# TensorE's program of a fused convolution and SwiGLU kernel: 28 written-out token tiles become a hardware loop over pairs of tiles

## The reference, cut to what matters

```python
def _attn_ref(x, weight_gen):               # x (4, 4096, 192), weight_gen (4, 4096, 8, 7)
    w = exp(weight_gen - max) ; w = w / (sum(w) + 1e-9)           # softmax over 7 taps
    x_unf = windows of 7 tokens of x, padded with 6 zero tokens in front
    return einsum('bshk,bskhg->bshg', w, x_unf)                   # 16384 tokens of 192

def _moe_ref(x, w_gate, w_val, w_out, rms_g):
    xn = x / sqrt(mean(x * x) + 1e-06) * rms_g
    g = xn @ w_gate                         # 192 x 1536
    silu = g * (1.0 / (1.0 + np.exp(-g)))
    val = xn @ w_val                        # 192 x 1536
    return (silu * val @ w_out)             # 1536 x 192
```

## Time and profile before

| | before |
|---|---|
| time, median of 3 (lowest, highest) | 1334.78 us (1332.74, 1336.92) |
| profiled execution, its own time | 1334.78 us |
| its span, first to last instruction | 1333.0 us |
| mean granted TensorE clock | 0.988 of full |
| TensorE busy, matmuls | 1280.2 us (96%), 13524 |
| VectorE busy | 995.2 us (75%) |
| ScalarE busy | 662.8 us (50%) |
| GpSimd busy | 97.1 us (7%) |

### The profile page before, as it was taken

How to read it: one execution, slowest core, us unless ns; L and a number is a source line. 1 busy time by engine, 2 the same in 40 slices (tenths; PEclk the granted TensorE clock), 3 DMA queues, 4 the chain that set the end, 5 groups by cost and what they waited for, 6 DMA issues and landing times.

```text
span 1333.0 us, 33644 instructions
## 1 busy us (share of the span) xinstructions
PE 1280.2 (96%) x13524; PEld 1230.0 (92%) x13524; DVE 995.2 (75%) x1438; ACT 662.8 (50%) x1427; POOL 97.1 (7%) x104
## 2 busy tenths in 40 slices
PE   3797899999999999999999999999999999999998
PEld 3686789999988889999999999999999999999998
DVE  6777867877777777777777777777777777777653
ACT  4364464455554455554445555445555544555543
POOL 7701200000000000000000000000000000000000
PEclk9798899999999999999999999999999999999999
DMA  9121111122112212212112211211221211121010
GB/s 306 35 67 25 50 58 55 37 67 67 49 60 64 57 37 66 66 43 66 54 40 63 66 58 51 66 55 37 66 66 43 66 55 52 52 66 34 16 37 13
DMA packets 20101, 77.69 MB, mean 58 GB/s; under 512 B 3215, under 2 KB 5007, under 8 KB 19854
## 3 DMA queue, kind: packets, MB, share of 16 engines
q1 hardware_dynamic: 19982, 75.83, 19.0%
HBM read 38.07 MB, written 12.58 MB: 38 GB/s over the span
## 4 chain that ended last, share of the span: by engine, by line
PE 91%; DVE 3%; ACT 2%; issue 2%; DMA 1%; POOL 0%; SPq 0%; POOLq 0%
PE up_ps L619 59%; PE out_ps L650 24%; PE out_ps L654 7%; DVE h L545 1%; DMA xT<-xT 1%; DVE prod L201 1%; PE up_ps L587 1%; DVE y L203 1%; ACT silu L422 0%; DVE tap_max L522 0%; ACT taps L403 0%; DVE h_lo L565 0%; ACT xn L386 0%; PE up_ps L591 0%; DMA taps<-in_weight_gen 0%
## 5 line engine op out<-in xcount | busy, mean ns | idle before, releaser
L619 PE MATMUL up_ps<-xT,w_hi 64*128 64x512 f32 x4608 | 823.3, 395 | 14.3 <-DVE h L545 6.8
L619 PEld LDWEIGHTS up_ps<-xT,w_hi 64*128 64x128 f32 x4608 | 540.2, 186 | 44.8 <-DMA xT<-xT 7.5
L619 PE MATMUL up_ps<-xT,w_lo 64*128 64x512 f32 x2304 | 521.8, 394 | 0.0
L650 PE MATMUL out_ps<-wo,h_hi 64*128 64x384 f32 x3072 | 468.4, 356 | 14.3 <-DVE h L545 12.6
L545 DVE TENSOR_TENSOR h<-up_ps,silu 128x512 f32<-128x512 f32 x384 | 264.9, 690 | 248.8 <-ACT silu L422 248.7
L654 PE MATMUL out_ps<-wo,h_lo 64*128 64x192 f32 x3072 | 433.6, 248 | 0.0
L429 ACT ACTIVATE h_hi<-h 128x512 fp32r<-128x512 f32 x384 | 242.7, 632 | 355.0 <-DVE h L545 355.0
L650 PEld LDWEIGHTS out_ps<-wo,h_hi 64*128 64x128 f32 x3072 | 370.7, 186 | 18.4 <-issue 14.9
L654 PEld LDWEIGHTS out_ps<-wo,h_lo 64*128 64x128 f32 x3072 | 372.9, 189 | 2.1
L422 ACT ACTIVATE silu<-up_ps 128x512 f32<-128x512 f32 x384 | 228.7, 596 | 274.9 <-PE up_ps L619 270.7
L619 PEld LDWEIGHTS up_ps<-xT,w_lo 64*128 64x128 f32 x2304 | 282.0, 186 | 12.9
(11 more groups left out here) (43 smaller groups left out, 315.2 us busy)
## 6 DMA issues: line engine op xcount, KB each, us to landing
x_buf<-in_x SPq DMA_DIRECT2D x30, 960.0 KB, 4.6
xT<-xT SPq DMA_DIRECT2D x96, 256.0 KB, 3.8
result<-last SPq DMA_DIRECT2D x32, 384.0 KB, 2.3
taps<-in_weight_gen SPq DMA_DIRECT2D x1, 3248.0 KB, 19.4
raw<-in_moe_w_gate SPq DMA_DIRECT2D x3, 384.0 KB, 6.4
raw<-in_moe_w_val SPq DMA_DIRECT2D x3, 384.0 KB, 7.5
last<-in_moe_w_out SPq DMA_DIRECT2D x1, 1152.0 KB, 12.4
x_first<-in_x SPq DMA_DIRECT2D x2, 384.0 KB, 4.9
```

The source lines that it names most:

```text
L619: mm = nc.tensor.matmul(ps[:, banks, :], w[rows, s, cols], xT[rows, t, s, part, :], start=(s == 0 and n == 0), stop=ends)
L650: nc.tensor.matmul(out_ps[:, j, 0:2 * D], h_hi[rows, g % HB, cols], wo[rows, g, :, :].rearrange("p a d -> p (a d)"), start=(g == 0 and k < ...
```

## The change

```diff
@@ -700,8 +700,10 @@
             turn_x(0, 0, 1)
             tile(0, 0, first=True)
             tile(1, 1)
-            for T in range(2, TILES - 1):
-                tile(T, T % 2)
+            with pe.Fori(1, TILES // 2 - 1) as i:
+                tile(2 * i, 0)
+                tile(2 * i + 1, 1)
+            tile(TILES - 2, 0)
             tile(TILES - 1, 1, last=True)
             project(TILES - 1, FB - 2)
```

## The result

| | before | changed |
|---|---|---|
| median of the runs timed together | 1334.94 us (1332.74 to 1336.92, 4 runs) | 1385.14 us (1381.82 to 1391.24, 4 runs) |
| ratio, 95% interval | | 1.0412 (1.0376 to 1.0448) |
| span of the profiled execution | 1333.0 us | 1382.9 us |
| mean granted clock | 0.988 | 0.983 |

The account below looks back on a forecast made before the run. The prediction took PE, gapless and busy 96% of the span, as the bound. Register steps 0, jump fetches 38 us and clock falls 13 us on 1334.8 us gave 1386 us, range 1350 to 1412.

Parts of the forecast that it names:

- The bound: Steady part: PE is busy 96% of the span with gapless matmuls, so each microsecond it stands still lengthens the time.
- Part 1: PE's loop body: 80 register steps, hidden behind matmuls, cost 0; upper bound 54 us.
- Part 2: The 13 jumps back: each idles PE 2.9 us for an instruction fetch, 38 us in all (22 to 52).
- The clock: Behind the jumps' idle: granted clock falls after two jumps in three, 1.5 us each, 13 us (0 to 20).
- The sum: Whole kernel: 1334.8 + 0 + 38 + 13 = 1386 us, 3.8% slower.
- the reason for the miss: At each jump: PE's program is streamed, not held, so the loop's head, seven packets back, must be fetched; chance 0.76.
- Rival A: At the jump back: the loop's head is still held, 0.3 us hides in the lead, 1334.8 us; chance 0.11.
- About as many instruction packets as before: Instruction queue: a sign of being right, the packet count staying near the kernel before's 108.
- B: Behind each jump: the second packet is not prefetched, so a second stall, 29 us more, 1415 us; chance 0.08.
- C: In `hidden` and `project`: register steps slow PE, 1389 us with jumps hidden, 1440 with both; chance 0.03.

Follow-up runs that it names:

- experiment 1: Changed kernel with all 28 tiles in one pass of the loop, so register steps but no jump back: 1334.83 us, ratio 0.9997 to the kernel before.
- experiment 3: Changed kernel with the loop rotated, so the jump back stands ahead of the odd tile's last `project`: 1361.1 us, ratio 1.0178.
- experiment 5: Kernel before, warm-up replaced by twelve unhinted loops, heads at packet start: jumps back 0.2 us up to 1782 instructions, 4.9 and 4.0 us at 2052.
- experiment 9: Changed kernel, no hint, with the loop's first instruction at place 0 of a packet: 1335.63 us, ratio 1.0001.
- experiment 10: Kernel before, warm-up replaced by eight unhinted loops, heads at place 0 or 128: jumps 0.2 us with seven packets touched; 1802 and 1682 instructions, eight packets, 3.5 to 4.
- experiment 4: Changed kernel with a prefetch hint for the loop's closing branch at the top of each pass: 1336.43 us, ratio 0.9996.
- experiment 8: Changed kernel, no hint, with the loop's first instruction at place 220 of a packet of 256: 1424.89 us, ratio 1.0668.

## Why the prediction was right, and where it was not

**The bound.** PE paced the steady part and no other engine could give time back: the idle time and the low clock together give the span's growth to within some 3 us, in three kernels with different shares of the two (accounts above).

**Part 1, register steps at 0.** Right, shown by experiment 1.

**Part 2, the size.** Predicted: a fetch of 3.5 us, 0.3 us of branch steps, a lead of 0.9, so 2.9 us of idle, 38 us in all. Measured: a branch of 3.61 us at the median, 0.3 us from its end to the first matmul (312.0 to 312.34), a lead of 0.7 (308.7 to the last matmuls around 309.4), and 40.0 us in 13 stretches, 3.1 us each. The middle between the two DMA rows came within 0.1 us of the branch, and that is partly luck: the packet itself starts 1.0 us into the branch and takes 1.0, and no row before said how the rest would be spent. The lead as a deduction is shown by experiment 3.

**The clock.** Predicted: nine falls of 1.5 us, 13 us; measured 7 us in the profiled execution, with a low level behind four stalls. This term was 6 us too large there. It is not steady: at the median clock of the 37 executions it is 14 us, and at the lowest, 0.968, some 26. Four tiles to a body lost 13 us with six stalls, five of them with a fall behind. Which stalls it falls after stays open.

**The sum.** 51 us predicted, 49.9 measured, with the idle a little over and the clock under. That the two cancel in this execution is luck; against the median of the 37 executions it is 51 for 55 us.

**The step that failed is the reason for the miss.** The prediction read the packets as "streamed, not held" and took a sequencer that "keeps only what is near". Experiments 5, 9 and 10 show that PE keeps seven packets behind a jump. The body has 1680 matmuls and weight loads and 109 others, 1789 instructions; from place 0 it fills seven packets all but three places. From any place above 3 it touches eight, as the changed kernel's must, and then nothing of that memory helps. Rival A got the point of decision right (the part of a packet ahead of the head, and the packet fetched in advance), and by it this kernel misses from all but four of the 256 places. So the forecast of a miss came true for a reason that it did not have, and there was luck in that: by the same reading, a body of 1522 instructions would have been forecast to miss as well, and it is at hand (experiment 10).

Why seven and not eight? With the hint PE keeps this same body although it touches eight (experiment 4), so there is room for eight. The instruction queue in the first pass of the changed kernel (135.4 to 225.5 us), and then in that of experiment 4 (135.4 to 226 us):

```profile
q8 instruction: 7, 0.11, 0.5%
...
q8 instruction: 6, 0.10, 0.5%
```

Six come at the same times in both, within 4 us. The seventh comes in the changed kernel alone, at 221.3 us, 4 us ahead of the first jump, as the last one did in the slow loop of experiment 10: it is the packet behind the loop, fetched in advance. A ninth packet in room for eight must take the place of one, and the oldest is the head's. The extra fetch is shown, and so is the missing head behind it; that the one overwrites the other is inferred.

The Trainium skill, "Runtime: NRT & Kernel Launch", section on instruction fetch mechanics, gives TensorE 128 KiB, 2048 instructions, in 16 KiB blocks. Experiments 4 and 10 agree with eight blocks of 256, by the working above. The same section lets a taken branch wait where its target is outside a window of two pages; for TensorE the runs differ, and the measurement decides: without a hint the target may be seven packets back, counting its own (experiments 5, 9 and 10).

**"About as many instruction packets as before".** Wrong: 138 against 108, 2.3 more for each jump. From the first branch to the last the changed kernel moves 117, nine in each pass: eight that the body touches and one in advance of the branch, which is not used. Written out, the same stretch moves 87. With the body held there are 21 in the whole kernel.

**Rivals B and C.** B did not happen in this kernel, and happens with the head at place 220 (experiment 8). Its condition, that the next packet is not fetched at once, is met in both kernels. C did not happen (experiment 1).

No version is faster than the kernel before: hint, placement and a single pass all tie with it. PE is the bound with or without the loop, and the loop can at best hide.

## What to carry to other kernels

Where an engine is gapless, ask of a loop on it how many instruction packets the body touches and how far the sequencer runs ahead at the jump. By experiments 5 and 10 a body of up to 1,537 instructions touches seven at most wherever its head lies, and one above 1792 never fits; between the two the place of the head decides. Where it does not fit, each jump back stalls for the branch's 3.6 us and the steps behind it, less that lead. A prefetch hint removes the stall at any of the lengths tried, a placed head only that of a body that fits seven packets; failing both, put the jump where the most work is queued. Compare such kernels with the head placed: the place alone separates 1336 us (place 0) from 1385 (where the code puts it) and 1425 (place 220).

## What the hardware showed that was not expected

A jump back of PE takes 0.21 us if the loop's body touches at most seven packets, and 3.3 to 4.9 us otherwise, with nothing in between (experiments 5 and 10; one entry branch, forward over the filling, took 2.3 us). With a hint of 31 ns at the top of the pass it takes 0.22 us for the bodies that are kept and 0.35 to 0.45 us for the two that are not (2052 instructions, and four tiles). A head late in its packet doubles the number of stalls (26 for 13 jumps), since the next packet starts only 2.3 to 3 us behind the branch there. With the body held, PE ran over 1,000 us without fetching one instruction packet, and that made it no faster than with the 87 of the kernel before.
